# A fused attention and two-layer feed-forward kernel: the first pair of heads scored straight from fp32 operands

## What is computed

```python
scores = scale * np.matmul(q, k.transpose(0, 1, 3, 2))      # q, k: (4, 8, 576, 64), scaled by about 31
mask = (rel >= 0) & (rel < 128)
scores = np.where(mask, scores + bias[None], -1000000000.0)
attn = np.exp(scores - np.max(scores, axis=-1, keepdims=True))
attn = attn / (np.sum(attn, axis=-1, keepdims=True) + 1e-09)
x = np.matmul(attn, v)                                      # then to (2304, 512)
...
h = x @ w_in        # 512 -> 2048, an activation, then @ w_out, 2048 -> 512; twice
```

## Time and profile before

| | |
|---|---|
| time, median of 3 runs | 856.89 us (856.84 to 856.97) |
| time of the profiled execution | 856.84 us |
| its span, first to last instruction | 855.1 us |
| PE busy | 847.5 us (99%) |
| DVE busy | 708.0 us (83%) |
| ACT busy | 536.8 us (63%) |
| POOL busy | 122.1 us (14%) |

### The profile page before, as it was taken

How to read it: one execution, slowest core, us unless ns; L and a number is a source line. 1 busy time by engine, 2 the same in 40 slices (tenths; PEclk the granted TensorE clock), 3 DMA queues, 4 the chain that set the end, 5 groups by cost and what they waited for, 6 DMA issues and landing times.

```text
span 855.1 us, 15514 instructions
## 1 busy us (share of the span) xinstructions
PE 847.5 (99%) x5746; PEld 844.0 (99%) x5746; DVE 708.0 (83%) x980; ACT 536.8 (63%) x789; POOL 122.1 (14%) x86
## 2 busy tenths in 40 slices
PE   8999999999999999999999999999999999999998
PEld 7999999999999999999999999999999999999998
DVE  7878896786988966778998897989989788889784
ACT  6788777767775536768644556767465567665441
POOL 4798898000000000000000000000000000000000
PEclk9999999999999999999999999999999999999999
DMA  8878761668676347686764762687647643788822
GB/s 202 221 201 224 205 171 67 263 241 288 249 252 228 129 149 271 247 309 243 259 245 177 282 237 108 218 282 260 230 145 277 226 152 125 289 300 294 308 74 75
DMA packets 63258, 186.45 MB, mean 218 GB/s; under 512 B 7505, under 2 KB 14353, under 8 KB 59345
## 3 DMA queue, kind: packets, MB, share of 16 engines
q1 hardware_dynamic: 62896, 185.30, 63.3%
q10 hardware_dynamic: 288, 0.16, 0.1%
HBM read 113.09 MB, written 72.35 MB: 217 GB/s over the span
## 4 chain that ended last, share of the span: by engine, by line
PE 96%; POOL 2%; DVE 1%; issue 1%; ACT 0%; POOLq 0%; DVEq 0%
PE ps L1068 83%; PE ps L1036 4%; PE ps L1002 3%; PE ps L1015 3%; PE ps L975 1%; POOL qk_hi L890 1%; POOL k_lo L886 1%; PE ps L1030 1%; PE ps L1045 1%; POOL arena L935 0%; DVE probs L1611 0%; DVE qk_hi L1587 0%; POOL wst L902 0%; PE ps L1050 0%; PE ps L1074 0%
## 5 line engine op out<-in xcount | busy, mean ns | idle before, releaser
L1068 PE MATMUL ps<-arena,w_first 128*128 128x384 f32 x1764 | 331.4, 336 | 0.0
L1068 PEld LDWEIGHTS ps<-arena,w_first 128*128 128x128 f32 x1764 | 310.8, 188 | 0.9 <-DVE arena L1718 0.5
L1068 PE MATMUL ps<-arena,w_rest 128*128 128x384 f32 x1260 | 240.3, 337 | 0.0
L1068 PEld LDWEIGHTS ps<-arena,w_rest 128*128 128x128 f32 x1260 | 220.2, 188 | 0.5 <-issue 0.3
L1718 DVE TENSOR_TENSOR arena<-raw_first,arena 128x768 fp32r<-128x768 f32 (+1 forms) x114 | 148.8, 1318 | 77.2 <-ACT arena L1311 77.2
L1311 ACT ACTIVATE arena<-raw_first 128x768 fp32r<-128x768 f32 (+1 forms) x120 | 132.0, 1118 | 45.5 <-DVE raw_first L1680 39.3
L1068 PE MATMUL ps<-w_rest,arena 128*128 128x256 f32 x945 | 132.4, 281 | 0.0
L1068 PEld LDWEIGHTS ps<-w_rest,arena 128*128 128x128 f32 x945 | 121.1, 189 | 0.1
L1068 PE MATMUL ps<-w_first,arena 128*128 128x256 f32 x567 | 88.0, 282 | 0.0
L1718 DVE TENSOR_TENSOR arena<-raw_rest,arena 128x1536 fp32r<-128x1536 f32 (+1 forms) x48 | 71.3, 1486 | 8.6 <-ACT arena L1311 8.4
L1068 PEld LDWEIGHTS ps<-w_first,arena 128*128 128x128 f32 x567 | 76.0, 189 | 0.0
(11 more groups left out here) (118 smaller groups left out, 972.6 us busy)
## 6 DMA issues: line engine op xcount, KB each, us to landing
gd<-g SPq DMA_DIRECT2D x24, 1536.0 KB, 6.2
raw_rest<-gd SPq DMA_DIRECT2D x32, 768.0 KB, 5.3
wst<-w_pairs SPq DMA_DIRECT2D x32, 512.0 KB, 5.7
raw_first<-gd SPq DMA_DIRECT2D x16, 768.0 KB, 6.1
yd<-ust SPq DMA_DIRECT2D x6, 1536.0 KB, 6.3
qk_raw<-qkT SPq DMA_DIRECT2D x30, 288.0 KB, 3.9
wd<-ust SPq DMA_DIRECT2D x4, 1536.0 KB, 9.1
raw_first<-yd SPq DMA_DIRECT2D x4, 1536.0 KB, 7.8
```

Of the source, the lines that this page charges most:

```text
L1068: last = nc.tensor.matmul(to, stationary, moving, start=start and n == 0, stop=n == len(steps) - 1, skip_group_check=True)
```

## The change

The first pair's scores are multiplied from `qk_raw` as it was loaded, as fp32 over 64 rows, one matmul for a block. Its roundings and subtractions, the second copy of its keys (four transfers), the 16 matmuls of zeros after m = 0, and eight of the 22 before it are gone. Head 4's load now waits until the fifth step's scores are done, since these read the raw slot itself (`last_use(0) + 1` is 5). The bias tables of the second pair are made after m = 2 instead of m = 3, the tail's table of the first pair after m = 1. DVE makes the low queries of heads 2 and 3 after m = 2 and m = 4 instead of directly behind their rounding. Two small strips of zeros are cleared besides. `splits` and `landings` count what the semaphores of the slots 0 and 1 now lack.

```diff
-WARM_UP = 22
-KEEP_WARM = 16
+WARM_UP = 14
...
-            sp.dma_start(piece(qk_raw, e, first)[UPPER], source_piece).then_inc(landed, 16)
-            sp.dma_start(piece_keys(qk_raw, e, first)[LOWER], source_keys).then_inc(landed, 16)
+            sp.dma_start(piece(qk_raw, e, first), source_piece).then_inc(landed, 16)
...
             if head - SPLIT_RING in (0, 1):
-                sp.wait_ge(first_split[slot], 2 - slot)
-            if head - SPLIT_RING == 1:
-                sp.wait_ge(first_keys_split, 1)
+
+                sp.wait_ge(scores_ready, last_use(head - SPLIT_RING) + 1)
...
-        split_first_keys()
-        split_rest_keys()
...
+        def first_scores(m):
+
+            d = ORDER[m][1]
+            if d == 2:
+                pe.wait_ge(cleared, CLEARED)
+                pe.wait_ge(first_in[0], 16)
+            elif d == 4:
+                pe.wait_ge(first_in[1], 16)
+            elif d == 3:
+                for head in (0, 1):
+                    pe.wait_ge(qk_in[head], landings(head))
+            wait_past(pe, scores_biased, m + 1 - SCORE_RING)
+            bank = score_bank[m % SCORE_RING]
+            for i, (e, blk) in enumerate(ITEMS[d] or ((0, 4), (1, 4))):
+                key0 = KEYS_AT[e] + (max(blk - 1, 0) * P if blk < 4 else SEQ - BAND)
+                query0 = QUERIES_AT[e] + blk * P if blk < 4 else TAIL_AT[e]
+                place = bank[:, i * BAND:(i + 1) * BAND] if d else bank[:, 0:BAND]
+                last = nc.tensor.matmul(place, qk_raw[UPPER, e, query0:query0 + P], qk_raw[UPPER, e, key0:key0 + BAND],
+                                        start=d > 0 or i == 0, stop=d > 0 or i == 1)
+            last.then_inc(scores_ready, 1)
...
-            if m < ALL_STEPS:
+            if m < STEPS:
+                first_scores(m)
+            elif m < ALL_STEPS:
                 scores(m)
-            if m == 0:
-                warm_up(KEEP_WARM)
-                pe.wait_ge(ident_in, 16)
...
-                if h == 0:
-                    round_first(1)
-                if pair == 0:
-                    round_rest(h)
...
-            if m in (3, 6, 11):
-                make_bias((3, 6, 11).index(m) + 1)
+            if m == 1:
+                act.wait_ge(tail_distance_in, 16)
+                make_tail_bias(0)
+            if m in (2, 6, 11):
+                make_bias((2, 6, 11).index(m) + 1)
+                make_tail_bias((2, 6, 11).index(m) + 1)
...
-        round_first()
         for m in range(ALL_STEPS + COPY_TAIL_LAG - 1):
...
-            if m == 0:
-                split_first_queries(1)
-                split_rest()
+            if m in (2, 4):
+                split_queries(m // 2 + 1)
             if m in (1, 2):
                 round_head(m + 1)
```

More of the change, by code:

```diff
@@ L86 @@
 CAST_LAG = (2, 2)
-CLEARED = 6
+CLEARED = 8
 SLOPES = tuple(2.0 ** (-8.0 * (h + 1) / HEADS) for h in range(HEADS))
@@ L175, in build @@
     first_in = [sem(f"first_in{e}") for e in range(2)]
[L176 to L180, removed]
     v_in = [sem(f"v_in{i}") for i in range(HEADS)]
@@ L277, in piece @@
     def piece(tile, e, first):
-        ap = tile[:, e]
+        ap = tile[UPPER, e]
         if e == 0:
@@ L284, in piece, with landings @@
         return ap[:, TAIL:keys_at] if first else ap[:, keys_at:WIDTH]
[L286 to L296, removed]
     def splits(head):
         use = head // SPLIT_RING
-        return 2 * use + 2 - (1 if head % SPLIT_RING == 1 else 0) if head >= 0 else 0
+        return 2 * use + 2 - (2 if head % SPLIT_RING < 2 else 0) if head >= 0 else 0
+    def landings(head):
+        return 32 * (head // SPLIT_RING + 1) - (16 if head % SPLIT_RING < 2 else 0)
     def last_use(head):
@@ L570, in load_piece @@
                 source_piece = qkT[1, :, 0:SEQ + FIRST_COLS] if first else qkT[1, :, SEQ + FIRST_COLS:2 * SEQ]
-            source_keys = qkT[e, :, SEQ * e:SEQ * (e + 1)]
-            source_keys = source_keys[:, 0:FIRST_COLS] if first else source_keys[:, FIRST_COLS:SEQ]
             landed = first_in[e] if first else qk_in[e]
-            sp.dma_start(piece(qk_raw, e, first)[UPPER], source_piece).then_inc(landed, 16)
-            sp.dma_start(piece_keys(qk_raw, e, first)[LOWER], source_keys).then_inc(landed, 16)
+            sp.dma_start(piece(qk_raw, e, first), source_piece).then_inc(landed, 16)
         def load_operands(head):
@@ L869, in _ @@
     def _(pool):
[L870 to L880, removed]
         def split_head(head):
@@ L978, in scores @@
             q, d = ORDER[m]
[L979 to L988, removed]
+            if d in (2, 3):
                 head = 2 * q if d == 2 else 2 * q + 1
@@ L1004, in scores @@
             last.then_inc(scores_ready, 1)
+        def first_scores(m):
[17 more added lines that the diff above has]
+            last.then_inc(scores_ready, 1)
         def transpose_probs(m):
             q, d = ORDER[m]
+            if m == 0:
+                pe.wait_ge(ident_in, 16)
             gi = group_of(m)
@@ L1221, in _ @@
         nc.scalar.activation(warm[:], warm[:], ACT.Exp).then_inc(warm_done, 1)
-        act.wait_ge(first_in[0], 32)
+        act.wait_ge(first_in[0], 16)
         act.dma_start(distance[:, BAND:], bias_table[:, BAND:]).then_inc(tail_distance_in, 16)
@@ L1244, in make_bias, with make_tail_bias @@
                 nc.scalar.activation(bias_sb[:, h], distance[:, 0:BAND], ACT.Copy, scale=SLOPES[h]).then_inc(bias_made, 1)
-                if h == 0:
-                    round_first(1)
-                if pair == 0:
-                    round_rest(h)
-            if pair == 0:
-                act.wait_ge(tail_distance_in, 16)
+        def make_tail_bias(pair):
             nc.scalar.activation(bias_tail[:, pair], distance[:, BAND:BAND + TAIL_KEYS], ACT.Copy,
                                  scale=SLOPES[2 * pair]).then_inc(bias_made, 1)
[L1254 to L1262, removed]
         def copy_pair(q):
@@ L1555, in _ @@
         for e in range(2):
+            nc.vector.memset(qk_raw[UPPER, e, ZEROS_AT[e]:ZEROS_AT[e] + TAIL], 0.0).then_inc(cleared, 1)
             nc.vector.memset(f32(qk_hi[:, e::2, ZEROS_AT[e]:ZEROS_AT[e] + TAIL]), 0.0).then_inc(cleared, 1)
         nc.vector.memset(half[:], 0.5).then_inc(cleared, 1)
[L1559 to L1580, removed]
         def round_head(head):
             slot, use = head % SPLIT_RING, head // SPLIT_RING
-            dve.wait_ge(qk_in[slot], 32 * (use + 1))
+            dve.wait_ge(qk_in[slot], landings(head))
             if use:
@@ L1587, in round_head, with split_queries @@
             nc.vector.tensor_copy(loaded(qk_hi, head), loaded(qk_raw, head)).then_inc(qk_rounded, 1)
[L1588 to L1591, removed]
+        def split_queries(head):
+            dve.wait_ge(qk_rounded, head - 1)
+            nc.vector.tensor_tensor(all_queries(qk_hi, head, LOWER), all_queries(qk_raw, head, UPPER),
+                                    f32(all_queries(qk_hi, head, UPPER)), ALU.subtract).then_inc(qk_split[head % SPLIT_RING], 1)
         def bias_scores(m):
```

## The result

The changed kernel takes 861.58 us (860.30 to 862.78, 6 runs) against 856.84 us (856.73 to 856.97, 6 runs) on the same chip: 4.7 us slower, ratio 1.0055 [1.0044, 1.0065]. The forecast was 854.4 us. The single runs of the changed kernel also lie 2.5 us apart, those of before 0.2. One execution among the later runs, at 1030.95 us and a clock of 0.752, belongs to the chip's slow state and is left out of its median.

The account below looks back on a forecast made before the run. PE was taken as the bound from 20 us on, so the start's gain carries to the end. The steps bring m = 11 2.5 us earlier: 856.9 - 2.5 = 854.4 us, range 853.2 to 856.9 us.

Parts of the forecast that it names:

- the clock: PE at the start: rises from 1.2 to 2.4 GHz at about 6.7 us and stays up despite later gaps.
- the slower rival: PE stays at 1.2 GHz under 64-row matmuls, m = 4 ends at 15.3 us: +1.8 us, 858.7 us, chance 0.12.
- The price of an fp32 matmul: First pair's scores on PE: two instructions per block at half column rate, 0.86 us a step instead of 0.48.
- Steps 1 and 2: First scores on PE: m = 0 starts at 4.5 instead of 6.26 us; m = 1 ends at 7.35, m = 2 at 8.2.
- Step 3: PE's transposes, m = 3 and m = 4 run without a wait, ending at 10.8 us, seen by others at 11.0.
- Steps 4 to 6: Head 4's load waits for m = 4, keeps 0.3 us; POOL starts at 16.15, m = 11 at 22.5 us.
- The size of the gain: m = 11 at 22.5 instead of 25.02 us, carried to the end: -2.5 us, chance 0.54.
- DVE's way to head 4: DVE reaches head 4 at about 13.9 us, waits for its transfer, and rounds it from 15.3 to 16.1 us.

Follow-up runs that it names:

- sixteen zeros put back: Changed kernel with the 16 matmuls of zeros after m = 0 restored; 861.57 us, ratio 1.0048.
- identity early: Changed kernel with the identity's load issued before ACT waits for the first piece; 861.86 us, ratio 1.0057.
- both mends: Changed kernel with fp32 scores over 128 rows (lower half zeros) and the identity loaded before ACT's wait for the first piece; 855.44 us, ratio 0.9985.
- run over 128 rows: Changed kernel with the same fp32 matmuls over 128 rows, lower half of both operands zero, identity still late; 858.18 us, ratio 1.0019.
- buffer of its own: Changed kernel with the first pair's raw operands in a separate buffer, so head 4's load waits for nothing; 861.51 us, ratio 1.0055.

## Why the prediction was wrong

It was wrong in sign. The step that failed is the clock: "Against it: PE stays busy from 1.36 to 9 us, and later gaps did not bring the clock down", with 0.12 for the slower rival.

1. **The price of an fp32 matmul** was right over 128 rows: four in 1.03 us with a tail of 0.39, or 0.215 us each. Over 64 rows, as in the change, one lasts as long (0.38 us, tail included), but a step with its transposes took 1.65 us instead of 1.35. The forecast has no term for that, and why it is so is not shown.
2. **Steps 1 and 2** were right in their times: m = 0 at 4.65 us, bias of m = 0 at 6.42 (forecast 4.5 and 6.5). The second is luck. The forecast had m = 0 at the low clock throughout; in the profiled execution the clock rose near 5 us. Where it stayed low, the four instructions took 2.07 us, not 1.8 (sixteen zeros put back), and the bias came at 7.05 (identity early).
3. **The clock.** PE was busy, but with matmuls over 64 rows. With the same zeros ahead and no gap, twelve of these from 4.65 us never raised the clock; over 128 rows it rose under them at about 6.5 us in one profile, and with both mends the kernel is 6.4 us quicker than over 64 rows. Zeros over 64 rows in the kernel before cost 2.2 us. I had read "busy" off the trace and not over how many rows. All the matmuls that preceded the rise in the kernel before, and those in the stretches with gaps, went over 128 rows. "Later gaps did not bring the clock down" was too weak as well: those gaps lay behind the sixteen zeros, and without these the granted clock is lower in all nine executions.
4. **Step 3, "No wait shows in between",** failed too. ACT issues the identity behind the first piece, and it took 4.6 us to land, not the 3.2 us of before. PE stood still in front of the first transposes, a wait that the sixteen zeros and the roundings had covered before. By itself that gap is not enough for the fall: in the profiled run over 128 rows PE is idle for 1.84 us and the clock holds. But five of the ten executions there list a lower clock and are slower, and with the gap gone none of ten. So rows and gap both count. In the profiled execution of the changed kernel the fall, at 8.7 us, lies within the gap.
5. **The slower rival** had the mechanism and was too cheap. It put m = 4's end at 15.3 us (15.24), head 4's landing at 19.6 (19.66), and m = 11 at 26.8, where 28.59 was measured. It let the clock matter only until head 4 had landed. It stayed low to 22.4 us and made PE the bound behind it as well: the sixteen value matmuls alone took 1.6 us more.
6. **Steps 4 to 6, the wait of head 4's load,** were not what decides. At the low clock it costs nothing (the buffer of its own gave 0.1 us against the changed kernel, whose executions lie 2.5 us apart, and 0.35 against the run with the identity early), with both mends nothing either; alone in the kernel before about 0.8 us, at the edge of what was measured.
7. **The size of the gain** was too large even with the clock held: 1.3 us instead of 2.5, m = 11 at 23.40 instead of 22.5. POOL's 6.3 us were right; it started head 4 at 17.04 us instead of 16.15. The mis-sized term is DVE's way to head 4, which the forecast had done at 13.9 us, waiting for the transfer at 15.3; it was done at 16.14 us, behind the transfer. Two things are in it. Head 2 landed at 9.60 us, 5.0 us from issue to landing, a time that the forecast does not name. And the low queries of heads 2 and 3 took 1.38 and 1.45 us beside POOL instead of 0.75, which I had put at nothing as hidden. That the landing is late because the loads are closer together is not shown; loading the values later did not help.

The Trainium skill ("TensorE: Matmul & The Clock Gate", Part 1) says that the clock monitor looks on its own rhythm, independent of a kernel's start. The scatter of single executions (860.30 to 862.78 us here, 856.22 to 862.05 over 128 rows with the gap) agrees with that, and so do the moments of the first rise behind the same 14 zeros (near 5 us in the changed kernel, 6.5 over 128 rows); no run here shows the rhythm itself.

What stays open is why the changed kernel's clock rose at all in the profiled execution near 5 us, and not before 23 us in the ones with the identity early and with the buffer of its own, whose PE work up to there is the same. One of the six executions of the changed kernel (861.03 us) also lists 1.000, as those two profiles do; that its clock never rose early is likely, not shown.

## What to carry to other kernels

Before work at the start of a kernel is thinned out, ask what keeps PE's clock up: read the rate of equal instructions, not the busy share and not the listed clock ahead of its first change, and see over how many rows the matmuls run. Here rows of zeros (64 cleared partitions) and an identity loaded earlier, together, turned a loss of 4.7 us into a gain of 1.3 us; the rows alone left a loss of 1.4 us, the identity alone one of 5.1. When a wait goes, list what its time had been covering: here it was the transfer of the identity. And a median can hide two kinds of executions; the clock listed for each sorts them.

## What the runs showed of the hardware

Matmuls over 64 rows lasted as long as over 128 rows: 22 zeros took 5.06 us at the low clock over either, and one fp32 instruction lasted 0.38 us at the high clock over either. Back to back from 1.36 to 10.1 us (14 zeros over 128 rows, then 12 fp32 instructions over 64) they left PE at 1.2 GHz in two profiles; in a third, of the changed kernel, the clock rose near 5 us with the same work ahead. In the kernel before, 22 and then 16 fp32r ones over 64 rows, with four scores over 128 rows between them, left it at 1.2 GHz up to 11 us. The clock also fell behind a wait of 1.13 us among matmuls over 128 rows (0.63 from 16 to 18 us), while behind a wait of 1.84 us in another kernel's execution it held. The granted clock is listed as 1.00 from the start of a profile until its first change, whatever the real level: the run with the identity early lists 1.00 throughout and issued at half rate until about 24 us.
